# Gate logits of the first mixture: from split operands over the whole array to full-precision matmuls in four column groups

## Chip, cores, metric

One core of a Trainium2 chip runs the whole program. The metric is the device time in microseconds (us) of one execution; the median of three runs is compared. Five engines work side by side, each with its own stream of instructions, and meet only in semaphores: TensorE (PE; its weight loads are shown as PEld), VectorE (DVE), ScalarE (ACT), GpSimd (POOL) and SyncE (SP, which only issues DMAs here).

## What is computed

```python
# attention without softmax, decaying with distance; q, k, v are (4, 8, 576, 64)
scores = (1 / sqrt(64)) * q @ k.T
x = (scores * Dmat) @ v                 # Dmat[i, j] = gamma_h ** (i - j) for j <= i
x = x.transpose(...).reshape(2304, 512)
# first mixture: all 8 experts for every token, weights from Sinkhorn
logits = x @ w_gate                     # (2304, 8)
P = exp(logits - logits.max()), 8 rounds of row and column normalisation
x = sum_e P[:, e] * (relu(x @ w1[e]) @ w2[e])
# second mixture: each token goes to its best expert alone
out = gate_w * (relu(x @ w1b[best]) @ w2b[best])
```

The change concerns `logits = x @ w_gate` of the first mixture. All that matters of it lies in the first 112 us.

## The kernel before

**Attention (0 to 97 us).** 24 chunks, numbered `n = 0..23` (4 batches `b` of `NC = 6` chunks `c` of 96 positions). For each, TensorE runs in this order: the scores of the next chunk (L1373), the state update K'V (L1389, left out for the last chunk of a batch), the product with the state (L1399, left out for the first), and the masked scores times V (L1404). VectorE masks the scores (`PT`, L923), ScalarE copies the state (`ST`, L703) and the chunk's output (`Xf`, L708), GpSimd applies the decays (`QT` L527, `VD` L533), SyncE loads `QK` and `KV` of chunk `n + 6` as soon as chunk `n` is done. All of it is plain fp32, and a plain fp32 matmul stands as two MATMUL records in the trace, with a weight load each. The output of a chunk goes to bank 4 for even `c` and bank 0 for odd `c` (`OB`).

**Gates.** `x` transposed lies in three tiles `Xf`, each of two halves of `W = 384` tokens. Such a half has its logits made as soon as its tokens are there, six gates in all; `GATES` has for each the tile, the half and the chunk that completes it. For the first five, ScalarE rounds the half to fp32r (`GH`, L792, behind that chunk), VectorE forms the rest (`GL`, L956, one chunk later), and TensorE multiplies `WGA`/`WGB` with them in 8 fp32r matmuls that fill the 128 columns of the array and accumulate in bank `RB` (L1423, L1424, behind chunk `n + 2`). VectorE then transposes the 32x384 result into `LX` (L964). The sixth gate (`last_gate`, L1432) multiplies the unsplit `Xf` with `wgp` (32 columns) in four plain fp32 matmuls accumulated in one column group, in the first step of the mixture.

**First mixture (from 97 us).** 96 steps `k`. In each, TensorE makes the hidden layer by a Winograd-like scheme of 7 products `p0..p6` (6 fp32r matmuls each, L1447 to L1451) and the output of the step before (L1470 to L1472). Operands: `XH`/`XL` (halves of x or its differences `Tf`), written by ScalarE (`x_hi`, L737) and VectorE (`x_lo`, L949); `W1H`/`W1L` and `W2H`/`W2L` by ScalarE (L720, L724) and GpSimd (L560, L565), in the first steps partly VectorE (L992, L999). The weights of a step arrive in one buffer, `w1raw`, so the load of step 1 waits until step 0's has been split (`s_w1l`) and summed (`Sf`, L553, `s_sum`). VectorE adds partial sums (`c12`, `c22`, `c21`: L1168 to L1183), and each next product waits for one of them.

What stands in the program behind chunk 21 on VectorE is an order written by hand in the loop over `n`; each engine does strictly what is next in its own stream.

Of the kernel before, what the change touches and what calls it, by code (L numbers as in the profile page):

```python
# [90 lines left out]
def build(nc, qk, kv, wg1, w11, w12, wg2, w21, w22, attn_tab, keep_tab, gate_rows, out):  # L91
    ctx = ExitStack()
    with ctx:
# [70 lines left out]
        GH, _ = place("GH", [P, ND, W], F32R, at_x + 3 * 4 * NK * W)  # L164
        GL, _ = place("GL", [P, ND, W], F32R, at_x + 8 * 4 * NK * W)
        WGA, a = place("WGA", [P, ND, P], F32R, at_raw + 4 * 4 * 2 * P)
        WGB, a = place("WGB", [P, ND, P], F32R, a)
        assert a == at_w1b
# [42 lines left out]
        causal = atab[0:C, o:o + C]  # L211
        wgraw, a = place("wgraw", [P, ND, E], F32, a)
# [118 lines left out]
        s_wgz, s_wgh, s_gh, s_gl, s_gate, s_lgt = (sem(f"s_{x}") for x in ("wgz", "wgh", "gh", "gl", "gate", "lgt"))  # L331
# [19 lines left out]
        OB = (4, 0)  # L351
# [29 lines left out]
        def _(sp):  # L381
# [53 lines left out]
            sp.wait_ge(s_gate, NG - 1)  # L435
# [260 lines left out]
        def _(act):  # L696
# [88 lines left out]
            def gate_hi(g):  # L785

                sb, half, n = GATES[g]
                act.wait_ge(s_x, 2 + n + 1)
                if g > 0:
                    act.wait_ge(s_gate, g)  # L790
                for a in (0, 2):
                    nc.scalar.activation(GH[:, a:a + 2, :], Xf[sb][:, a:a + 2, half, :], ACT.Copy).then_inc(s_gh, 1)  # L792

            for n in range(B * NC):
                chunk(n // NC, n % NC)
                if n == 2:
                    act.wait_ge(s_wgz, 2)
                    act.wait_ge(s_wg1, 16)
                    for t in (WGA, WGB):
                        nc.scalar.activation(t[:, :, 0:E], wgraw[:, :, :], ACT.Copy).then_inc(s_wgh, 1)  # L800
                if n == 20:
                    w1_hi(0, 0, 0)
                    w1_hi(0, 0, 1)
                for g in range(NG - 1):
                    if n == GATES[g][2]:
                        gate_hi(g)
                if n in (14, 16, 18):
                    x_hi(0, n // 2 - 7)
                if n == 22:
                    w1_hi(0, 0, 2)  # L810
                    act.wait_ge(s_gate, NG - 1)
                    x_hi(0, 3)
                    x_hi(0, 4)

            def step(k, q, first=False, last=False, sb=0, route=None, late_x=None, scale=None, tile=None):
# [39 lines left out]
                for i in range(1, 4):  # L855
                    hidden_hi(k, i)

# [43 lines left out]
        def _(dve):  # L901
# [10 lines left out]
            for t in (WGA, WGB, wgp):  # L912
                nc.vector.memset(t[:, :, :].bitcast(F32), 0.0).then_inc(s_wgz, 1)
# [37 lines left out]
            def gate_lo(g):  # L951

                sb, half, _ = GATES[g]
                for i, a in enumerate((0, 2)):
                    dve.wait_ge(s_gh, 2 * g + i + 1)
# [12 lines left out]
            mask(0, 0)  # L968
            for n in range(B * NC):
                if n < B * NC - 1:  # L970
                    mask(n + 1, (n + 1) % NC)
                if n == 3:
                    dve.wait_ge(s_wgh, 2)
                    nc.vector.tensor_tensor(WGA[:, :, E:2 * E], wgraw[:, :, :], WGA[:, :, 0:E].bitcast(F32),
                                            ALU.subtract).then_inc(s_wgh, 1)
                    dve.wait_ge(s_wgz, 3)
                    nc.vector.tensor_copy(wgp[:, :, 0:E], wgraw[:, :, :]).then_inc(s_wgh, 1)
                for g in range(NG - 1):
                    if n == GATES[g][2] + 1:
                        gate_lo(g)  # L980
# [5 lines left out]
                if n in (15, 17, 19):  # L986
                    x_lo(0, (n - 15) // 2, s_xlp if n == 19 else s_xl)
# [15 lines left out]
            x_lo(0, 3, s_xlp)  # L1003
            x_lo(0, 4, s_xlp)
# [208 lines left out]
            def step(sb, k, e, q, **at):  # L1213
# [151 lines left out]
        def _(pe):  # L1365
# [48 lines left out]
            def gate(g):  # L1414

                sb, half, _ = GATES[g]
                if g == 0:
                    pe.wait_ge(s_wgh, 4)
                else:
                    pe.wait_ge(s_lgt, g * P // SQ)  # L1420
                pe.wait_ge(s_gl, 2 * g + 2)
# [3 lines left out]
                last.then_inc(s_gate, 1)  # L1425

            def last_gate():

                pe.wait_ge(s_lgt, (NG - 1) * P // SQ)
                sb, half, _ = GATES[NG - 1]  # L1430
                for a in range(ND):
                    last = mm(bank[RB][0:SQ, 0:W], wgp[:, a, :], Xf[sb][:, a, half, :],  # L1432
                              start=(a == 0), stop=(a == ND - 1))
# [7 lines left out]
            pe.wait_ge(s_x, 2 + B * NC)  # L1441
# [144 lines left out]
            for sb in range(SB):  # L1586
                for j in range(NQ if sb == 0 else PEEL * NQ):
# [3 lines left out]
                    if k == 0:  # L1591
                        after[7] = last_gate
# [105 lines left out]
```

## Time and profile before

| | us |
|---|---|
| median of 3 runs | 1906.84 (1906.82 to 1907.41) |
| the profiled execution | 1912.71 |
| its span, first to last instruction | 1911.1 |
| PE busy | 1887.9 (99%) |
| DVE busy | 1194.2 (62%) |
| POOL busy | 1085.7 (57%) |
| ACT busy | 633.5 (33%) |
| mean granted TensorE clock | 0.994 |

The profiled execution is 5.9 us above the median of the runs; differences between two places in the trace are taken as they are. A row of the timeline gives start, duration, engine, line, operation, tiles and shapes, how often it is repeated, and in square brackets how long the engine sat idle before and what ended that. Matmul durations include the pipeline, so what a matmul costs is read from one start to the next.

### The profile page before, as it was taken

What the parts mean: (1) busy time and instruction counts of PE and PEld (TensorE: products, weight loads), DVE (VectorE), ACT (ScalarE), POOL (GpSimd) and SP (SyncE); (2) the same over time, 40 slices, a digit from 0 to 9 for tenths busy, and PEclk for the clock granted to TensorE, in tenths of its full rate; (3) what the DMA queues carried; (4) which work ended last, traced back from release to release, by engine and by line L of the source; (5) the groups of instructions that cost most, each with busy time, mean ns of one, the idle gap of its engine ahead of it and who ended that gap; (6) DMA issues with size and microseconds to landing.
All of it is one profiled execution on the core that took longest, in us unless ns stands there. A gap on an engine that the chain in (4) does not pass through costs nothing.

```text
span 1911.1 us, 31124 instructions
## 1 busy us (share of the span) xinstructions
PE 1887.9 (99%) x11118; PEld 1709.1 (89%) x11118; DVE 1194.2 (62%) x2177; ACT 633.5 (33%) x1107; POOL 1085.7 (57%) x910
## 2 busy tenths in 40 slices
PE   8999999999999999999999999999999999999997
PEld 7889989999999999999999999999999999999997
DVE  4786765555567777775556777878666665322533
ACT  2543343333334333333333433333333332101221
POOL 5766666666678666666667876766666653111111
PEclk9999999999999999999999999999999998999999
DMA  9724444454444212122112122212222213312742
GB/s 232 185 95 149 155 155 155 148 165 158 153 161 140 67 67 83 67 83 66 66 66 78 66 78 74 87 67 78 78 99 99 88 61 122 138 35 67 266 175 69
DMA packets 123956, 212.16 MB, mean 111 GB/s; under 512 B 8974, under 2 KB 58126, under 8 KB 123856
## 3 DMA queue, kind: packets, MB, share of 16 engines
q1 hardware_dynamic: 118816, 195.31, 31.6%
q0 software_dynamic: 5040, 15.51, 2.4%
q8 instruction: 63, 1.03, 0.2%
q14 instruction: 37, 0.30, 0.1%
HBM read 162.65 MB, written 49.19 MB: 111 GB/s over the span
## 4 chain that ended last, share of the span: by engine, by line
PE 96%; DMA 1%; DVE 1%; issue 0%; SPq 0%; ACT 0%; POOL 0%; POOLq 0%; DVEq 0%; ACTq 0%
PE bank L1471 14%; PE bank L1472 14%; PE bank L1470 14%; PE bank L1447 12%; PE bank L1451 12%; PE bank L1449 12%; PE bank L1619 8%; PE bank L1629 2%; PE bank L1630 2%; PE bank L1631 2%; DMA wgraw<-in_moe_w_gate 1%; PE bank L1373 1%; PE bank L1404 1%; PE bank L1399 1%; PE bank L1583 1%; PE bank L1389 0%
## 5 line engine op out<-in xcount | busy, mean ns | idle before, releaser
L1210 DVE SCALAR_TENSOR_TENSOR acc<-bank,Pw,acc 128x512 f32<-128x512 f32 x516 | 386.1, 751 | 233.7 <-PE bank L1472 221.8
L1472 PE MATMUL bank<-W2H,HL 128*128 128x512 f32 x1152 | 450.1, 391 | 0.0
L1471 PE MATMUL bank<-W2L,HH 128*128 128x512 f32 x1152 | 450.0, 391 | 0.0
L1470 PE MATMUL bank<-W2H,HH 128*128 128x512 f32 x1152 | 449.2, 390 | 0.0
L560 POOL TENSOR_TENSOR W1L<-w1raw,W1H 128x512 fp32r<-128x512 f32 (+1 forms) x190 | 192.2, 1034 | 339.1 <-ACT W1H L720 339.1
L1447 PE MATMUL bank<-XHa,W1H 128*128 128x384 f32 x960 | 321.4, 335 | 2.0 <-DVE c L1183 1.1
L1451 PE MATMUL bank<-XHa,W1L 128*128 128x384 f32 x960 | 321.1, 334 | 0.0
L1449 PE MATMUL bank<-XLa,W1H 128*128 128x384 f32 x960 | 321.0, 334 | 0.0
L743 ACT ACTIVATE HH<-c 128x384 fp32r<-128x384 f32 x288 | 150.4, 526 | 489.5 <-PE bank L1472 324.5
L1472 PEld LDWEIGHTS bank<-W2H,HL 128*128 128x128 f32 x1152 | 216.2, 188 | 45.3
L1471 PEld LDWEIGHTS bank<-W2L,HH 128*128 128x128 f32 x1152 | 216.2, 188 | 42.8
L1470 PEld LDWEIGHTS bank<-W2H,HH 128*128 128x128 f32 x1152 | 216.3, 188 | 42.4
L565 POOL TENSOR_TENSOR W2L<-w2raw,W2H 128x1024 fp32r<-128x1024 f32 x96 | 230.5, 2402 | 27.2 <-ACT W2H L724 27.1
L560 POOL TENSOR_TENSOR W1L<-Sf,W1H 128x1024 fp32r<-128x1024 f32 x94 | 225.6, 2400 | 0.0
L553 POOL TENSOR_TENSOR Sf<-w1raw 128x256 f32<-128x256 f32 x192 | 147.7, 769 | 127.4 <-DMA w1raw<-in_moe_w 121.8
L743 ACT ACTIVATE HH<-bank 128x384 fp32r<-128x384 f32 x96 | 47.1, 491 | 447.7 <-PE bank L1472 447.7
L1188 DVE SCALAR_TENSOR_TENSOR HL<-c,HH 128x384 fp32r<-128x384 f32 x288 | 176.6, 620 | 11.0
L1447 PEld LDWEIGHTS bank<-XHa,W1H 128*128 128x128 f32 x960 | 180.2, 188 | 3.4 <-issue 1.7
L1451 PEld LDWEIGHTS bank<-XHa,W1L 128*128 128x128 f32 x960 | 180.2, 188 | 0.0
L1449 PEld LDWEIGHTS bank<-XLa,W1H 128*128 128x128 f32 x960 | 180.2, 188 | 0.0
L1619 PEld LDWEIGHTS bank<-x2T,Wa 128*128 128x128 f32 x1408 | 163.4, 194 | 1.9
L1619 PE MATMUL bank<-x2T,Wa 128*128 128x128 f32 x1408 | 164.3, 278 | 0.0
(198 smaller groups left out, 2616.6 us busy)
## 6 DMA issues: line engine op xcount, KB each, us to landing
w1raw<-in_moe_w SPq DMA_DIRECT2D x96, 512.0 KB
w2raw<-in_moe_w SPq DMA_DIRECT2D x96, 512.0 KB
sorted_rows<-blank SPq DMA_DIRECT2D x147, 257.0 KB, 3.7
Wa<-in_moe_w SPq DMA_DIRECT2D x7, 2048.0 KB, 7.5
Wb<-in_moe_w SPq DMA_DIRECT2D x7, 2048.0 KB, 9.8
QK<-qk SPq DMA_DIRECT2D x24, 384.0 KB, 8.4
KV<-kv SPq DMA_DIRECT2D x24, 384.0 KB, 9.7
nxt<-sorted_rows POOLq DMA_DIRECT2D x23, 257.0 KB
```

The lines of the kernel that those rows point to most:

```text
L560: nc.gpsimd.tensor_tensor(W1L[s][:, blk, :], raw, W1H[s][:, blk, :].bitcast(F32), ALU.subtract).then_inc(s_w1l, 1)
L565: nc.gpsimd.tensor_tensor(W2L[s][:, :, :], w2raw[:, :, :], W2H[s][:, :, :].bitcast(F32), ALU.subtract).then_inc(s_w2l, 1)
L743: nc.scalar.activation(HH[:, i, :], source, ACT.Relu).then_inc(s_hhi, 1)
L1188: nc.vector.scalar_tensor_tensor(HL[:, i, :], source, 0.0, HH[:, i, :].bitcast(F32), ALU.max, ALU.subtract).then_inc(s_hlo, 1)
L1210: ins = nc.vector.scalar_tensor_tensor(tile, psum, weight, tile, ALU.mult, ALU.add)
L1447: mm(bank[b][:, 0:W], W1H[s][:, blk, :], XH[i][:, c, :], start=start and c == 0, stop=False, skip_group_check=True)
L1449: mm(bank[b][:, 0:W], W1H[s][:, blk, :], XL[i][:, c, :], start=False, stop=False, skip_group_check=True)
L1451: last = mm(bank[b][:, 0:W], W1L[s][:, blk, :], XH[i][:, c, :], start=False, stop=(c == NK - 1), skip_group_check=True)
L1470: mm(dst, HH[:, h, tok], W2H[s][:, m, :], start=(m == 0), stop=False)
L1471: mm(dst, HH[:, h, tok], W2L[s][:, m, :], start=False, stop=False)
L1472: last = mm(dst, HL[:, h, tok], W2H[s][:, m, :], start=False, stop=(m == 1))
L1619: last = mm(bank[HB[j // 4]][:, (j % 4) * P:(j % 4 + 1) * P], Wa[s][:, a, j * P:(j + 1) * P], x2T[:, a, :], start=(a == 0), stop=(a == ND ...
```

## The change

The first five gates lose their split: no `GH`, `GL`, `WGA`, `WGB`. All six gates use the unsplit `Xf` and `wgp`, one plain fp32 matmul for each of the four blocks of 128 features, each into 32 partitions of its own of bank `RB`, so that each uses 32 of the array's columns. VectorE adds the four partial results: copies partitions 64 to 127 to `GS`, adds them onto 0 to 63, copies 32 to 63, adds them onto 0 to 31, each waiting for the one before, and then transposes as it did. For the last gate ScalarE makes the two copies (`GS_last`). The chunks' output banks are swapped, so that the last chunk writes bank 4, and TensorE no longer waits for its copy before the first product, which writes bank 0. The operand parts 3 and 4 of `x` are made behind chunks 19 and 21 instead of behind the loop. SyncE's load of the first `w2` no longer waits for the fifth gate.

```diff
-            OB = (4, 0)
+            OB = (0, 4)
@@ SyncE
-            sp.wait_ge(s_gate, NG - 1)
             load_w2(0, 0)
@@ ScalarE
-            def gate_hi(g): ...
-                    nc.scalar.activation(GH[:, a:a + 2, :], Xf[sb][:, a:a + 2, half, :], ACT.Copy).then_inc(s_gh, 1)
             for n in range(B * NC):
                 chunk(n // NC, n % NC)
...
-                if n in (14, 16, 18):
-                    x_hi(0, n // 2 - 7)
+                if n in (14, 16, 18, 19, 21):
+                    x_hi(0, (14, 16, 18, 19, 21).index(n))
                 if n == 22:
                     w1_hi(0, 0, 2)
-                    act.wait_ge(s_gate, NG - 1)
-                    x_hi(0, 3)
-                    x_hi(0, 4)
@@ ScalarE, step 0 of the mixture
                 for i in range(1, 4):
                     hidden_hi(k, i)
+                    if fixed(k, 0) and i == 1:
+                        act.wait_ge(s_gate, NG)
+                        nc.scalar.activation(GS_last[:, :], bank[RB][2 * SQ:P, 0:W], ACT.Copy).then_inc(s_gs, 1)
+                if fixed(k, 0):
+                    act.wait_ge(s_gsum, 1)
+                    nc.scalar.activation(GS_last[0:SQ, :], bank[RB][SQ:2 * SQ, 0:W], ACT.Copy).then_inc(s_gs, 1)
@@ VectorE
-            def gate_lo(g): ...
-                    nc.vector.tensor_tensor(GL[:, a:a + 2, :], Xf[sb][:, a:a + 2, half, :],
-                                            GH[:, a:a + 2, :].bitcast(F32), ALU.subtract).then_inc(s_gl, 1)
             def gate_tokens(g):
                 dve.wait_ge(s_gate, g + 1)
+                if g < NG - 1:
+                    link(nc.vector.tensor_copy(GS[:, :], bank[RB][2 * SQ:P, 0:W]))
+                    link(nc.vector.tensor_tensor(bank[RB][0:2 * SQ, 0:W], bank[RB][0:2 * SQ, 0:W], GS[:, :], ALU.add))
+                    link(nc.vector.tensor_copy(GS[0:SQ, :], bank[RB][SQ:2 * SQ, 0:W]))
+                    link(nc.vector.tensor_tensor(bank[RB][0:SQ, 0:W], bank[RB][0:SQ, 0:W], GS[0:SQ, :], ALU.add))
+                else:
+                    dve.wait_ge(s_gs, 2)
+                    link(nc.vector.tensor_tensor(bank[RB][0:SQ, 0:W], bank[RB][0:SQ, 0:W], GS_last[0:SQ, :],
+                                                 ALU.add))
...
-                if n in (15, 17, 19):
-                    x_lo(0, (n - 15) // 2, s_xlp if n == 19 else s_xl)
+                if n in (15, 17, 19, 20, 22):
+                    x_lo(0, (15, 17, 19, 20, 22).index(n), s_xl if n < 19 else s_xlp)
...
                     w1_sums_lo(1)
+                    dve.wait_ge(s_gs, 1)
+                    nc.vector.tensor_tensor(bank[RB][0:2 * SQ, 0:W], bank[RB][0:2 * SQ, 0:W], GS_last[:, :],
+                                            ALU.add).then_inc(s_gsum, 1)
@@ TensorE
             def gate(g):
...
                 for a in range(ND):
-                    mm(bank[RB][:, 0:W], WGA[:, a, :], GH[:, a, :], start=(a == 0), stop=False)
-                    last = mm(bank[RB][:, 0:W], WGB[:, a, :], GL[:, a, :], start=False, stop=(a == ND - 1))
+                    last = mm(bank[RB][SQ * a:SQ * a + SQ, 0:W], wgp[:, a, :], Xf[sb][:, a, half, :],
+                              start=True, stop=True)
                 last.then_inc(s_gate, 1)
...
-            pe.wait_ge(s_x, 2 + B * NC)
+            pe.wait_ge(s_x, 1 + B * NC)
```

VectorE's stream before, from the transposes of the fourth gate (behind the mask of chunk 21) to those of the fifth:

```order
L964 STREAM_TRANSPOSE LX<-bank 32x96 x4
L923 TENSOR_TENSOR PT_107<-bank,atab 96x384 x2
L956 TENSOR_TENSOR GL<-Xf_66,GH 128x768 x2
L992 TENSOR_TENSOR W1L_50<-w1raw,W1H_49 128x512
L992 TENSOR_TENSOR W1L_50<-w1raw,W1H_49 128x256
L923 TENSOR_TENSOR PT_109<-bank,atab 96x384 x2
L999 TENSOR_TENSOR W1L_50<-Sf,W1H_49 128x1024
L949 TENSOR_TENSOR XLa<-Xf_64,XHa 128x768
L949 TENSOR_TENSOR XLa<-Tf,XHa 128x768
L964 STREAM_TRANSPOSE LX<-bank 32x96 x4
```

The same stretch of VectorE's stream in the changed kernel (its own line numbers), from the fourth gate's sums on; those of the fifth gate stand behind the last row:

```order
L938 COPY GS<-bank 64x384
L939 TENSOR_TENSOR bank<-bank,GS 64x384
L940 COPY GS<-bank 32x384
L941 TENSOR_TENSOR bank<-bank,GS 32x384
L947 STREAM_TRANSPOSE LX<-bank 32x96 x4
L931 TENSOR_TENSOR XLa<-Xf_64,XHa 128x768
L905 TENSOR_TENSOR PT_104<-bank,atab 96x384 x2
L971 TENSOR_TENSOR W1L_50<-w1raw,W1H_49 128x512
L971 TENSOR_TENSOR W1L_50<-w1raw,W1H_49 128x256
L905 TENSOR_TENSOR PT_106<-bank,atab 96x384 x2
L931 TENSOR_TENSOR XLa<-Tf,XHa 128x768
L978 TENSOR_TENSOR W1L_50<-Sf,W1H_49 128x1024
```

The `GL` pair ahead of the first split of `w1raw` is gone; four sums stand ahead of the transposes, one operand part ahead of the mask of chunk 22 and one behind that of chunk 23.

VectorE's stream in step 0 of the mixture before, from the split of the weight sums of step 1 on:

```order
L999 TENSOR_TENSOR W1L_52<-Sf,W1H_51 128x1024
L1188 SCALAR_TENSOR_TENSOR HL<-c_75,HH 128x384
L1181 TENSOR_TENSOR c_74<-c_74,bank 128x384
L1183 TENSOR_TENSOR c_76<-cs_73,bank 128x384
L1188 SCALAR_TENSOR_TENSOR HL<-c_74,HH 128x384
```

The same place in the changed kernel:

```order
L978 TENSOR_TENSOR W1L_52<-Sf,W1H_51 128x1024
L1216 TENSOR_TENSOR bank<-bank,GS_last 64x384
L1165 SCALAR_TENSOR_TENSOR HL<-c_75,HH 128x384
L1158 TENSOR_TENSOR c_74<-c_74,bank 128x384
L1160 TENSOR_TENSOR c_76<-cs_73,bank 128x384
L1165 SCALAR_TENSOR_TENSOR HL<-c_74,HH 128x384
```

One sum of the last gate now stands between that split and `c21` (`c_76`).

## Rows read from the trace of the kernel before

**Rows 1.** The page's part 4, the chain that ended last.

```profile
PE 96%; DMA 1%; DVE 1%; issue 0%; SPq 0%; ACT 0%; POOL 0%; POOLq 0%; DVEq 0%; ACTq 0%
```

**Rows 2.** Waits of PE, 8 to 110 us: total, times, longest.

```profile
PE bank L1389 <- issue: 1.8, 2, 1.3
PE bank L1399 <- issue: 1.8, 2, 1.0
...
PE bank L1447 <- ACT Xf L708: 0.8, 1, 0.8
PE bank L1404 <- DVE PT L923: 0.4, 1, 0.4
```

**Rows 3.** Stretches between PE's stalls: length, PE busy (records), clock, DMA share, GB/s.

```profile
29.61:37.12 7.51, 7.51 (x127) 1.00 1.04 236
...
54.42:61.78 7.36, 7.34 (x126) 1.00 1.03 242
```

**Rows 4.** DMA queues, 29 to 63 us: packets, MB, share of the engines.

```profile
q8 instruction: 4, 0.07, 0.9%
```

**Rows 5.** Timeline of PE where it resumes after the first and the last such stall.

```profile
38.44 0.50 PE L1389 MATMUL bank<-VD,KV 96*64 96x64 f32 x9 [1.32 <-issue]
...
62.55 0.40 PE L1399 MATMUL bank<-QT,ST 64*64 64x96 f32 x5 [0.78 <-issue]
```

**Rows 6.** Timeline of PE: last product ahead of the third gate, its first matmul, what follows it.

```profile
69.06 0.88 PE L1404 MATMUL bank<-PT,VD 96*64 96x96 f32 x16
69.87 0.44 PE L1423 MATMUL bank<-GH,WGA 128*128 128x384 f32 x1
...
71.46 0.92 PE L1373 MATMUL bank<-QT,QK 64*96 64x96 f32 x16
```

**Rows 7.** Timeline of PE: the last gate, what follows, and step 1's second product.

```profile
103.16 2.77 PE L1432 MATMUL bank<-Xf,wgp 128*32 128x384 f32 x8
105.85 0.44 PE L1447 MATMUL bank<-XHb,W1H 128*128 128x384 f32 x1
...
110.02 0.41 PE L1447 MATMUL bank<-XHa,W1H 128*128 128x384 f32 x1 [0.76 <-DVE c L1183]
```

**Rows 8.** A stretch: length, PE, PEld, DVE, ACT, POOL busy, clock, DMA share, GB/s.

```profile
39.20:42.50 3.30, 3.30 (x40) 2.85 (x38) 0.00 (x0) 1.03 (x3) 1.00 (x2) 0.50 1.04 242
```

**Rows 9.** Timeline of DVE: two operations with a link behind, and a copy from a bank.

```profile
115.92 0.69 DVE L1204 COPY acc<-bank 128x512 f32<-128x512 f32 x1 [0.32 <-PE bank L1472]
...
129.74 0.32 DVE L1028 TENSOR_TENSOR bank<-bank,cs 128x144 f32<-128x144 f32 x1
130.09 0.32 DVE L1041 TENSOR_REDUCE bank<-bank 128x18 f32<-128x144 f32 x1
```

**Rows 10.** Timeline of DVE, 85 to 110 us.

```profile
85.76 1.18 DVE L964 STREAM_TRANSPOSE LX<-bank 32x96 f32<-32x96 f32 x4
...
89.15 2.88 DVE L956 TENSOR_TENSOR GL<-Xf,GH 128x768 fp32r<-128x768 f32 x2 [0.23 <-ACT GH L792]
91.96 3.09 DVE L992 TENSOR_TENSOR W1L<-w1raw,W1H 128x512 fp32r<-128x512 f32 x2
94.97 1.01 DVE L923 TENSOR_TENSOR PT<-bank,atab 96x384 f32<-96x384 f32 x2
...
97.90 0.95 DVE L949 TENSOR_TENSOR XLa<-Tf,XHa 128x768 fp32r<-128x768 f32 x1
...
105.33 3.15 DVE L999 TENSOR_TENSOR W1L<-Sf,W1H 128x1024 fp32r<-128x1024 f32 x1
...
109.33 0.54 DVE L1183 TENSOR_TENSOR c<-cs,bank 128x384 f32<-128x384 f32 x1
```

**Rows 11.** Timeline of POOL: step 0's last weight sum, step 1's first, its `W2L`.

```profile
93.59 1.18 POOL L553 TENSOR_TENSOR Sf<-w1raw,Sf 128x256 f32<-128x256 f32 x1
98.74 0.74 POOL L553 TENSOR_TENSOR Sf<-w1raw 128x256 f32<-128x256 f32 x1 [3.97 <-DMA w1raw<-in_moe_w]
...
105.01 2.39 POOL L565 TENSOR_TENSOR W2L<-w2raw,W2H 128x1024 fp32r<-128x1024 f32 x1
```

More of the change, by code:

```diff
@@ L163, in build @@
         assert 4 * 6 * D <= RSTEP and a + 4 * D <= at_h
[L164 to L168, printed above, removed]
+        GS, _ = place("GS", [2 * SQ, W], F32, at_c + 3 * 4 * W)
         KV, QK = [], []
@@ L211, in build @@
         causal = atab[0:C, o:o + C]
+        GS_last, g_end = place("GS_last", [2 * SQ, W], F32, a - 4 * attn_tab.shape[1])
+        assert g_end <= a
         wgraw, a = place("wgraw", [P, ND, E], F32, a)
@@ L330, in build @@
         s_dve = sem("s_dve")
-        s_wgz, s_wgh, s_gh, s_gl, s_gate, s_lgt = (sem(f"s_{x}") for x in ("wgz", "wgh", "gh", "gl", "gate", "lgt"))
+        s_wgz, s_wgh, s_gate, s_lgt, s_gs, s_gsum = (sem(f"s_{x}") for x in ("wgz", "wgh", "gate", "lgt", "gs", "gsum"))
         s_mx, s_gmx, s_nmx, s_exp = sem("s_mx"), sem("s_gmx"), sem("s_nmx"), sem("s_exp")
@@ L784, in _ @@
             act.wait_ge(s_x, 2)
[L785 to L791, printed above, removed]
-                    nc.scalar.activation(GH[:, a:a + 2, :], Xf[sb][:, a:a + 2, half, :], ACT.Copy).then_inc(s_gh, 1)
             for n in range(B * NC):
                 chunk(n // NC, n % NC)
[L796 to L800, printed above, removed]
                 if n == 20:
@@ L803, in _ @@
                     w1_hi(0, 0, 1)
-                for g in range(NG - 1):
-                    if n == GATES[g][2]:
-                        gate_hi(g)
-                if n in (14, 16, 18):
-                    x_hi(0, n // 2 - 7)
+                if n in (14, 16, 18, 19, 21):
+                    x_hi(0, (14, 16, 18, 19, 21).index(n))
                 if n == 22:
                     w1_hi(0, 0, 2)
-                    act.wait_ge(s_gate, NG - 1)
-                    x_hi(0, 3)
-                    x_hi(0, 4)
             def step(k, q, first=False, last=False, sb=0, route=None, late_x=None, scale=None, tile=None):
@@ L911, in _ @@
             nc.vector.memset(ST[0][:, 1, :], 0.0).then_inc(s_x, 1)
-            for t in (WGA, WGB, wgp):
-                nc.vector.memset(t[:, :, :].bitcast(F32), 0.0).then_inc(s_wgz, 1)
+            nc.vector.memset(wgp[:, :, :], 0.0).then_inc(s_wgz, 1)
             dve.wait_ge(s_atab, 16)
@@ L949, in x_lo @@
                 nc.vector.tensor_tensor(XL[i], part, XH[i].bitcast(F32), ALU.subtract).then_inc(done, 1)
[L951 to L955, printed above, removed]
-                    nc.vector.tensor_tensor(GL[:, a:a + 2, :], Xf[sb][:, a:a + 2, half, :],
-                                            GH[:, a:a + 2, :].bitcast(F32), ALU.subtract).then_inc(s_gl, 1)
             def gate_tokens(g):
@@ L972, in _ @@
                 if n == 3:
[L973 to L976, printed above, removed]
+                    dve.wait_ge(s_wgz, 1)
+                    dve.wait_ge(s_wg1, 16)
                     nc.vector.tensor_copy(wgp[:, :, 0:E], wgraw[:, :, :]).then_inc(s_wgh, 1)
                 for g in range(NG - 1):
-                    if n == GATES[g][2] + 1:
-                        gate_lo(g)
                     if n == GATES[g][2] + 3 and n < B * NC - 1:
@@ L1002, in _ @@
             w1_sums_lo(0)
-            x_lo(0, 3, s_xlp)
-            x_lo(0, 4, s_xlp)
             gate_tokens(NG - 2)
@@ L1414, in gate @@
             def gate(g):
-                sb, half, _ = GATES[g]
                 if g == 0:
-                    pe.wait_ge(s_wgh, 4)
+                    pe.wait_ge(s_wgh, 1)
                 else:
                     pe.wait_ge(s_lgt, g * P // SQ)
-                pe.wait_ge(s_gl, 2 * g + 2)
+                sb, half, n = GATES[g]
+                pe.wait_ge(s_x, 2 + n + 1)
                 for a in range(ND):
-                    mm(bank[RB][:, 0:W], WGA[:, a, :], GH[:, a, :], start=(a == 0), stop=False)
-                    last = mm(bank[RB][:, 0:W], WGB[:, a, :], GL[:, a, :], start=False, stop=(a == ND - 1))
[L1425 to L1433, printed above, removed]
+                    last = mm(bank[RB][SQ * a:SQ * a + SQ, 0:W], wgp[:, a, :], Xf[sb][:, a, half, :],
+                              start=True, stop=True)
                 last.then_inc(s_gate, 1)
@@ L1591, in _ @@
                     if k == 0:
-                        after[7] = last_gate
+                        after[7] = (lambda: gate(NG - 1))
                     if k == 1:
```

## The prediction, made before the changed kernel had run

> **What bounds the kernel now.** The chain that ended last is PE for 96% [rows 1]. So what the first 110 us gain or lose on PE shifts all the rest, and I ask only when PE passes a late point there: the second product of step 1, at 110.02 [rows 7]. The waits of PE say what holds it before that. The reader is to see that they are few: 1.8 and 1.8 us of "issue", 0.8 for the last chunk's copy, 0.4 for a mask [rows 2].
>
> The "issue" waits matter most. They cut a group of like matmuls in two (x9 and x5 are the remainders of groups of 16 [rows 5]), where the code has no wait. The stretches from one to the next hold 127 and 126 MATMUL records [rows 3], with as many weight loads some 256 instructions, whatever they are. The DMA queue "instruction" moved four packets in 29 to 63 us [rows 4], in which there are four such stalls (two of each line [rows 2]), while the engines of the DMA were at 1.03 to 1.04 [rows 3]. I read this as PE running out of instructions: the next 256 are asked for when the present ones begin, and come late behind the loads of QK and KV. Then up to 62.55 the pace is that of these fetches, and PE work saved inside such a stretch only lengthens its stall. After 62.55 there is no such stall.
>
> The other chain ends at `w1raw`. VectorE's `GL` (2.88 us from 89.15) stands ahead of its first split, which ends at 95.05 [rows 10]; then step 1's `w1raw` is loaded (POOL idle 3.97 us until 98.74 [rows 11]), summed, split, and after VectorE's split of the sums (105.33 to 108.48) and `c21` PE resumes at 110.02, having waited 0.76 [rows 7, 10].
>
> **The gate on PE.** Before, 8 fp32r matmuls: 71.46 - 69.87 = 1.59 us [rows 6]. After, 4 plain fp32 matmuls, 8 records. In one column group these 8 take 105.85 - 103.16 = 2.69, or 0.336 each [rows 7]: that is the upper bound. The masked product runs in two groups of 64 columns: 16 records of 96 columns would be 16 x 0.336 x 96/384 = 1.34 one after another, and took 69.87 - 69.06 = 0.81 [rows 6]. So two groups do overlap. With four at once two records' time is left, 0.67, and I add 0.11 for the change of form: 0.78, the lower bound. If they overlap only in pairs, four records' time: 1.45. I take 0.78, since nothing in the rows of two groups shows a limit. Saved per gate: 0.81; by pairs 0.14; without overlap 1.10 lost.
>
> The Trainium skill ("TensorEngine Tiling (Array Packing)", section Theoretical Speedup) gives up to 4 times for 32 columns, and the trace agrees for two groups. Its section PSUM Bottleneck on that page speaks against the change: after such a speedup the copy out of PSUM may become the bottleneck. By that rule VectorE's sums would set the pace; the terms for them follow from rows.
>
> **Which gates count.** Gates 0 (behind chunk 5) and 1 (behind chunk 11) lie before 62.55, in stretches that end in a stall; their 0.81 goes into it. Gates 2 and 3 lie behind: 2 x 0.81 = 1.62 sooner, everything from chunk 20 on. Call it X.
>
> **VectorE's sums.** A copy of 512 columns from a bank takes 0.69, an in-place multiply of 144 in a bank 0.32 [rows 9]: about 1.0 ns a column, so 384 columns 0.56. With a link the next starts 130.09 - 129.74 = 0.35 after a start, 0.03 over its duration. Four sums: 4 x 0.59 = 2.4 us. In front of the last mask (94.97 before) go 2.88 of `GL` and the idle time; what comes is 2.4 and one part of x (0.95, as the like row). Laid end to end from 85.76: sums to 88.2, transposes to 89.3, x part to 90.3, mask to 91.2, split of `w1raw` (3.03, of which I assume nothing is saved) to 94.2, mask to 95.2 [rows 10]. So the split ends 0.8 sooner than 95.05, besides X. Bounds for the four: 1.4 (0.35 each) and 2.8 (0.69 each); both keep the split ahead of POOL's sums, next.
>
> **The load of `w1raw`.** It needs VectorE's split and POOL's sums, which end at 94.77 [rows 11] and whose pace PE sets. So it comes at 94.8 - X, 0.3 better than X alone. The sums, splits and `W2L` behind it move along: `W2L`, which ended at 107.40, at 107.1 - X. VectorE's split of the sums took 3.15 and ended 1.08 after `W2L` [rows 10, 11], as if it got nowhere beside it; again it ends 1.08 behind, 108.2 - X. VectorE gets there in time even though the fifth gate's sums delay `c12` and `c22`: laid out as above its queue is free for it at 105.6 - X, with PE idle some 2.5 us in step 0. Here the last gate's shortening (2.69 to 0.78) goes: PE is sooner and waits longer.
>
> **The added sum ahead of `c21`.** 0.59, with nothing beside it, then as before 1.4 from the split's end (108.48) to `c21` (109.87) and 0.15 to PE: 110.3 - X. Against 110.02: +0.3 - 1.62 = -1.3.
>
> **At nothing.** ScalarE loses `GH` and gains two copies of about half a microsecond behind work that PE needs only eight matmul groups later. The first product no longer waits 0.8 for the last chunk's copy [rows 2]; it starts sooner, and the time is spent again at 110. The parts 3 and 4 of x on ScalarE lie in its idle time. The load of `w2` stands in SP's queue behind `w1raw`'s, which is issued after the fifth gate anyway. Without that cover each would cost up to its own 0.5 to 1 us.
>
> **Sum.** Against its own execution 1912.7 - 1.3 = 1911.4 (span 1909.8). The median of the runs is 5.9 lower, so 1906.84 - 1.3 = 1905.5.
>
> **Rivals.**
> *The clock falls.* After the 1.32 us stall before 38.44 the granted clock was 0.50 over 39.20 to 42.50, 1.2 instead of 2.4 GHz [rows 5, 8]; after the stalls of 1.0 and 0.78 it stayed at 1.00 [rows 2, 3]. The change lengthens idle time: the stall before 62.55 from 0.78 to 1.6, and PE now has 2.5 in step 0 and about 2 before 110, in place of 0.76. A fall costs half of 3.3 us, 1.65, where PE is the bound: one gives 1907.2, two 1908.8. Three, or one that lasts longer, give 1910.4 and more: slower. The point to pass is one more stall as long as the 1.32 us after which it fell. For it: the stalls grow beyond that. Against it: part of the slow time lies ahead of waits and is hidden.
> *Full saving.* If the "issue" stalls are not fetches, gates 0 and 1 count too: -2.9, 1903.9; if the fall at 39.2 also goes, 1902.3, faster. Against it: the 127, 127 pattern.
> *No overlap, or in pairs.* Column groups of one bank, with four moving operands of 128 rows, may share a path. In pairs X = 0.3: 1906.8. Not at all: gates 2 and 3 lose 2.2, gate 1 its 1.1 less the 0.8 stall: X = -2.5, 1909.6. Two groups overlapping speaks against it.
> *The change does nothing here*, as the gates' saving and VectorE's cost cancel: 1906.8, no other than pairs.
>
> **How the numbers follow.** A measurement of this kernel tells about 0.2%, 3.8 us, from no change: below 1903.0 is faster, over 1910.7 slower. Chances: the sum 0.34; one or two falls 0.25; three or a long one (slower) 0.10; full saving 0.09, with more than that (faster) 0.10; pairs or none 0.12, of which 0.03 slower with a fall. So faster 0.10, same 0.77, slower 0.13. The range leaves out the slower tail and the fastest: 1903.0 to 1909.8.
>
> **What would show it.** Right: a gate of 0.7 to 0.9 us from start to start; no `GH`/`GL`; still stalls each 127 records up to about 62.5, the ones before 38.4 and 62.5 longer by 0.8; four sums at 0.59; PE idle over 1.5 us before the second product of step 1, now near 108.7, on `c21`. Wrong: scores of chunk 17 sooner by more than 0.8, a gate over 1.2, a clock of 0.50 anywhere in 60 to 115, or PE waiting for a mask more than 0.5 us.

## The result, and the profile after

| us | before | after |
|---|---|---|
| median (six runs each) | 1906.83 (1901.57 to 1907.79) | 1914.01 (1912.61 to 1918.18) |
| the profiled execution, span | 1912.71, 1911.1 | 1913.54, 1911.9 |

After against before: 1.0039, interval [1.0023, 1.0054]: slower, by some 7 us, and above the predicted range. The same kernel run again later gave 1.0049 [1.0036, 1.0063]. The two profiled executions differ by only 0.8 us, so a single pair of traces would have hidden the result: before's happens to be 6 us above its median, after's is at its own. The two were also 2.7 us apart before the first gate ran, after the same work on PE: the masked product ahead of it starts at 28.56 in after and at 31.27 in before, whose early waits are 1.1 us longer (5.6 against 4.5 us from 8 to 28 us) and which has a stretch at half clock there. That part of after's lead is no effect of the change. Three lines of before: its longest wait, that stretch (0.50 is the clock), and the product.

```profile
PE bank L1373 <- POOL QT L527: 4.3, 2, 3.4
...
11.80:15.20 3.40, 3.40 (x46) 3.10 (x48) 0.87 (x2) 2.32 (x4) 1.99 (x2) 0.50 1.03 230
...
31.27 0.88 PE L1404 MATMUL bank<-PT,VD 96*64 96x96 f32 x16
```

The page of after. PE has less to do (1882.2 against 1887.9) and is yet later.

```profile
PE 1882.2 (98%) x11118; PEld 1700.8 (89%) x11118; DVE 1195.0 (63%) x2186; ACT 627.1 (33%) x1097; POOL 1086.0 (57%) x910
...
PE 95%; DVE 2%; POOL 1%; issue 1%; DMA 1%; ACT 0%; SPq 0%; POOLq 0%; DVEq 0%; ACTq 0%
```

The waits of PE in after, 8 to 111 us (total, times, longest); they answer to [rows 2]. The copy of the last chunk is gone from the list. New are 3.7 us on `c21` (L1160) and 2.3 for a mask (L905).

```profile
PE bank L1419 <- DVE c L1160: 3.7, 1, 3.7
PE bank L1353 <- POOL QT L524: 2.8, 2, 2.5
PE bank L1384 <- DVE PT L905: 2.6, 2, 2.3
PE bank L1369 <- issue: 1.7, 2, 1.0
PE bank L1419 <- DVE c L1151: 1.4, 1, 1.4
PE bank L1353 <- issue: 1.2, 1, 1.2
```

The timeline of PE in after: the second gate with what follows it, then the place where PE waits for the mask of chunk 14, and the third gate.

```profile
49.42 0.85 PE L1404 MATMUL bank<-Xf,wgp 128*32 128x384 f32 x8
50.20 0.92 PE L1353 MATMUL bank<-QT,QK 64*96 64x96 f32 x16
...
60.33 1.39 PE L1384 MATMUL bank<-PT,VD 96*64 96x96 f32 x14 [2.33 <-DVE PT L905]
...
67.34 1.51 PE L1404 MATMUL bank<-Xf,wgp 128*32 128x384 f32 x8
68.78 1.43 PE L1353 MATMUL bank<-QT,QK 64*96 64x96 f32 x16
```

A gate takes 50.20 - 49.42 = 0.78 us, as predicted. The third takes 1.44, because it ran at half the clock, as these stretches of after show (length, busy times, clock, DMA share, GB/s):

```profile
59.60:69.80 10.20, 9.47 (x100) 7.28 (x102) 3.49 (x7) 2.47 (x5) 4.00 (x4) 0.50 0.58 167
110.80:114.20 3.40, 3.40 (x13) 3.40 (x12) 2.88 (x8) 3.35 (x7) 2.58 (x3) 0.51 0.00 0
121.10:124.50 3.40, 3.40 (x10) 2.63 (x9) 1.02 (x3) 0.25 (x1) 1.42 (x3) 0.50 0.00 0
```

Why the mask is late stands in VectorE's timeline of after, just ahead:

```profile
51.43 1.01 DVE L905 TENSOR_TENSOR PT<-bank,atab 96x384 f32<-96x384 f32 x2
52.46 0.56 DVE L938 COPY GS<-bank 64x384 f32<-64x384 f32 x1
...
54.82 1.19 DVE L947 STREAM_TRANSPOSE LX<-bank 32x96 f32<-32x96 f32 x4
56.04 1.59 DVE L924 TENSOR_TENSOR Tf<-Xf 128x768 f32<-128x768 f32 x1
57.55 1.79 DVE L924 TENSOR_TENSOR Tf<-Xf,Tf 128x768 f32<-128x768 f32 x1
59.27 1.94 DVE L905 TENSOR_TENSOR PT<-bank,atab 96x384 f32<-96x384 f32 x4
```

Between two masks stand four sums (54.82 - 52.46 = 2.36 us), four transposes and two differences `Tf`: 59.27 - 52.46 = 6.8 us. PE idles 2.33 us for the second mask, and from 59.6 to 69.8 the granted clock is 0.50. In before the same place took 63.22 - 59.37 = 3.85 us:

```profile
59.37 1.18 DVE L964 STREAM_TRANSPOSE LX<-bank 32x96 f32<-32x96 f32 x4
...
63.22 1.01 DVE L923 TENSOR_TENSOR PT<-bank,atab 96x384 f32<-96x384 f32 x2
```

VectorE and GpSimd of after around step 1's second product; they answer to [rows 10, 11].

```profile
97.97 0.74 POOL L550 TENSOR_TENSOR Sf<-w1raw 128x256 f32<-128x256 f32 x1 [5.22 <-DMA w1raw<-in_moe_w]
...
104.44 2.38 POOL L562 TENSOR_TENSOR W2L<-w2raw,W2H 128x1024 fp32r<-128x1024 f32 x1 [0.18 <-ACT W2H L721]
...
114.68 2.39 POOL L562 TENSOR_TENSOR W2L<-w2raw,W2H 128x1024 fp32r<-128x1024 f32 x1 [0.22 <-ACT W2H L721]
117.03 2.42 POOL L557 TENSOR_TENSOR W1L<-Sf,W1H 128x1024 fp32r<-128x1024 f32 x1
```

```profile
105.25 2.66 DVE L978 TENSOR_TENSOR W1L<-Sf,W1H 128x1024 fp32r<-128x1024 f32 x1
107.83 0.55 DVE L1216 TENSOR_TENSOR bank<-bank,GS_last 64x384 f32<-64x384 f32 x1
108.30 1.08 DVE L1165 SCALAR_TENSOR_TENSOR HL<-c,HH 128x384 fp32r<-128x384 f32 x1
109.30 0.54 DVE L1158 TENSOR_TENSOR c<-c,bank 128x384 f32<-128x384 f32 x1
109.77 0.54 DVE L1160 TENSOR_TENSOR c<-cs,bank 128x384 f32<-128x384 f32 x1
...
114.79 2.45 DVE L989 TENSOR_TENSOR lg<-LX 128x144 f32<-128x144 f32 x1
117.27 0.30 DVE L990 TENSOR_REDUCE mx<-lg 128x1 f32<-128x144 f32 x1
117.61 1.92 DVE L991 TENSOR_SCALAR diag<-ktab,mx 128x128 f32<-128x128 f32 x1
```

PE of after at the same place: the second product of step 1, and the `diag` matmul.

```profile
110.45 0.41 PE L1419 MATMUL bank<-XHa,W1H 128*128 128x384 f32 x1 [3.69 <-DVE c L1160]
...
119.58 0.49 PE L1504 MATMUL bank<-diag,ktab 128*128 128x128 f32 x2 [1.77 <-DVE diag L991]
```

The same three operations in before, ahead of GpSimd's `W2L` or just clear of it:

```profile
113.55 0.31 DVE L1012 TENSOR_TENSOR lg<-LX 128x144 f32<-128x144 f32 x1
...
114.23 0.32 DVE L1014 TENSOR_SCALAR diag<-ktab,mx 128x128 f32<-128x128 f32 x1
```

```profile
114.49 2.41 POOL L565 TENSOR_TENSOR W2L<-w2raw,W2H 128x1024 fp32r<-128x1024 f32 x1
```

The second product starts at 110.45 against 110.02: 0.4 later, though the first product started 4.3 sooner (93.43 against 97.75). From there on: 1.7 us for the clock at 110.8, 1.77 of wait for `diag`, 1.7 for the clock at 121.1; with the 0.4 that is 5.6 us. The shift measured is 5.4: one and the same VectorE operation, the 1500th from the end, starts at 1078.11 and at 1072.72. Near 1609 before's profile has 10.2 us at half the clock, with PE busy and not one wait, which after's lacks, and 0.8 is left at the end.

**How the clock is weighed over many runs.** Each timed run lists its span and its mean granted clock; span x (1 - clock) is the time lost at half clock. As a mean over the runs it is 7.3 to 8.0 us for before (four sets of 23 to 35 runs) and 13.1 and 14.1 for after (6 and 6). Span x clock, the time at full clock, is 1896.6 to 1897.2 against 1900.0 and 1900.4. So 5 to 7 us of the loss are clock and some 3 are not. I call the first "clock loss" below. The scatter of the runs leaves such a mean uncertain by some 0.5 us for a set of before, 1 for twelve runs and up to 2 for five or six, so differences of 1 to 2 us in it mean little.

### The profile page after: what moved, and what is told of

The parts are those of the page before. It is cut to its first block, busy times and chain, and to the rows that moved or that the text cites. A ratio compares the mean times of both kernels' runs of the same rounds, so it can differ in the third digit from the quotient of the medians.

```text
span 1911.9 us, 31121 instructions
## 1 busy us (share of the span) xinstructions
PE 1882.2 (98%) x11118; PEld 1700.8 (89%) x11118; DVE 1195.0 (63%) x2186; ACT 627.1 (33%) x1097; POOL 1086.0 (57%) x910
## 4 chain that ended last, share of the span: by engine, by line
PE 95%; DVE 2%; POOL 1%; issue 1%; DMA 1%; ACT 0%; SPq 0%; POOLq 0%; DVEq 0%; ACTq 0%
PE bank L1443 14%; PE bank L1444 14%; PE bank L1442 14%; PE bank L1419 12%; PE bank L1423 12%; PE bank L1421 12%; PE bank L1591 8%; PE bank L1602 2%; PE bank L1601 2%; PE bank L1603 2%; PE bank L1384 1%; PE bank L1353 1%; PE bank L1379 1%; PE bank L1555 1%; PE bank L1369 0%
```

## The experiments

All are timed against the kernel before on the same chip; each ratio is against it. Where two variants are compared with each other, some 3 us (0.15%) is what their intervals leave open. Not one leaves out part of the computation; some add work whose result is not used.

**The last gate as before.** After, but with the old `last_gate` (one column group) and no sums for it.

```diff
-    mm(bank[RB][SQ * a:SQ * a + SQ, 0:W], wgp[:, a, :], ..., start=True, stop=True)
+    mm(bank[RB][0:SQ, 0:W], wgp[:, a, :], ..., start=(a == 0), stop=(a == ND - 1))
... (without the copies to GS_last on ScalarE and its sums on VectorE)
```

> The changed kernel, but with the last gate as before: four matmuls accumulated in one column group (2.69 us of PE), no copies by ScalarE and no sums by VectorE for it. Theory A (the loss is made in steps 0 and 1: VectorE's added sums push c21 and the diagonal behind GpSimd's operations, PE idles 3.7 and 1.8 us, and the clock falls to half twice): the wait for the diagonal (1.77) goes, the wait ahead of step 1's second product shrinks from 3.69 to about 1.8 less 0.6, at most one fall is left, and the time is 1914.0 less 4 to 5.5: 1908.5 to 1910, or 1907 with no fall at all. Theory B (the loss comes from the attention stage: the 2.33 us wait for a mask and the 10 us at half clock behind it): no gain, 1913 to 1915.

1911.28, 1.0029 [1.0017, 1.0041]; clock loss 13.2, full-clock time 1896.6. No wait for `diag`, 2.7 us on `c21`, still 2.3 for the mask. The time lies between what the two theories wanted. So the last gate holds perhaps 2.7 us, within what the intervals leave open, and the larger part is elsewhere.

**The diagonal later.** After, with TensorE's `diag` matmuls two output groups on.

```diff
-                        after["t0"] = diagonal
+                        after["t2"] = diagonal
```

> The changed kernel, with the matmul on the diagonal issued behind the third output tile of step 1 instead of the first. Theory A: PE no longer waits 1.77 us there, and the fall of the clock behind that wait (3.4 us at half, 1.7 us lost) goes with it: 1914.0 - 3.5 = 1910.5. Theory B (attention stage): 1914. If only the wait goes and the clock falls all the same: 1912.3.

1914.17, 1.0046 [1.0033, 1.0059]. The wait for `diag` is gone from the profile, the full-clock time is 1896.2, but the clock loss is 16.5: nothing won, against theory A.

**Filling the wait.** After, with 16 matmuls (results unused) ahead of step 1's second product.

```diff
+                    if fixed(k, 1):
+                        for i in range(16):
+                            mm(bank[7][:, 0:W], W1H[s][:, 0, :], XH[0][:, 0, :], start=True, stop=True)
```

> The changed kernel, with 16 matmuls more (128x384, fp32r, about 2.8 us, results unused, in a bank that is free) behind the first product of step 1, where PE waits 3.69 us for c21. They add work inside a wait. If the clock falls at 110.8 because PE idled before it (theory A), the wait shrinks to about 0.9, the clock stays at full speed there, and the time falls by 1.7: 1912.3, with the second wait for the diagonal unchanged or up to 1.7 longer, since PE is there sooner. If idling has nothing to do with the fall: 1914.

1913.38, 1.0042 [1.0029, 1.0056]; clock loss 11.1. PE waits 0.9 in place of 3.7 and its profile has no fall at 110 and one alone, of 3.4 us, at 60.2. But this profile is of the quickest of the five runs (1906.74; the others 1912.37 to 1915.73), and the median is what it was. That the falls behind 110 cost nothing is not shown by it, as five runs would not show 1.7 us.

**The late mask removed.** After, with the third and fourth difference `Tf` one chunk later, so that they no longer stand with the second gate's sums ahead of one mask.

```diff
-                if n in (11, 12):
-                    x_term(0, 2 * n - 22)
-                    x_term(0, 2 * n - 21)
+                if n in (11, 13):
+                    x_term(0, n - 11)
+                    x_term(0, n - 10)
```

> The changed kernel, with VectorE's third and fourth difference of x moved from behind chunk 12's place in its stream to behind chunk 13's, so that the mask of chunk 14 does not stand behind them and the second gate's four sums. Theory A: PE's wait of 2.33 us at 58 and the 10.2 us at half clock behind it go, PE is at the mixture up to 5 us sooner, and the whole comes out at 1913 to 1914 all the same, because the load of the weights of step 1 hangs on the landing of those of step 0 and PE waits longer. Theory B: 1914.0 less up to 7: 1907 to 1909.

1909.81, 1.0019 [1.0007, 1.0032]; clock loss 11.1: 4.2 us given back, the largest effect of one edit. PE no longer waits there, and no fall of the clock stands between 43 and 107 us in the profile. Theory A, no gain, is out. VectorE there, with a mask now between transposes and differences:

```profile
57.21 1.19 DVE L947 STREAM_TRANSPOSE LX<-bank 32x96 f32<-32x96 f32 x4
58.43 1.02 DVE L905 TENSOR_TENSOR PT<-bank,atab 96x384 f32<-96x384 f32 x2
59.37 0.95 DVE L924 TENSOR_TENSOR Tf<-Xf 128x768 f32<-128x768 f32 x1
60.23 0.95 DVE L924 TENSOR_TENSOR Tf<-Xf,Tf 128x768 f32<-128x768 f32 x1
61.10 1.01 DVE L905 TENSOR_TENSOR PT<-bank,atab 96x384 f32<-96x384 f32 x2
```

**Both.** The last gate as before and the late mask removed.

> The changed kernel with both of the single edits: last gate as before (4.0 to 2.7 us better than the change in the runs so far) and VectorE's differences of x one chunk later (4.2 us better). If the two losses are separate (the mask wait with its falls of the clock; the last gate's sums ahead of c21 and the diagonal): 1914.0 - 2.7 - 4.2 = 1907.1, no difference from before that can be told. If they are one and the same loss met twice (falls of the clock that come wherever PE idles): 1909 to 1911, with a mean clock still under that of before.

1906.80, 1.0003 [0.9991, 1.0015]; clock loss 9.1, full-clock time 1896.0. The two effects add up (1914.0 - 2.7 - 4.2 = 1907.1), and with them the whole loss is gone, with the first five gates still in column groups. Against the kernel with the old last gate alone the late mask is worth 1911.3 - 1906.8 = 4.5. Nothing is won either, as far as can be told: the 1.3 us that I had predicted lie inside this interval.

**Single parts, from the kernel before.** Only the banks swapped, and only the first five gates in column groups (sums with them, the parts of `x` where they were, SyncE's wait gone). The edit of the first:

```diff
-            OB = (4, 0)
+            OB = (0, 4)
-            pe.wait_ge(s_x, 2 + B * NC)
+            pe.wait_ge(s_x, 1 + B * NC)
```

> The kernel before, with only the output banks swapped and the wait for the last chunk's copy gone. PE starts the mixture 0.8 us sooner and waits 0.8 us longer for c21 of step 0, which hangs on the weights' load: theory A (the load chain sets the end of step 0) 1906, unchanged. If PE set it: 1905.1. If the longer wait there already brings a fall of the clock: 1907.7.

> The kernel before, with only the first five gates changed (full precision, four column groups, VectorE's four sums) and SyncE's wait for them gone; last gate, banks and the operand parts 3 and 4 as before. Theory A2 (the gates' sums make the mask of chunk 14 late, PE waits 2.3 us and the clock falls; the mixture's part of the loss is the last gate's): about 4 us over before, 1910, with a mean clock lower than before by about 0.002. If the loss is all in the last gate and the moved parts: 1905 to 1906.

Banks: 1906.38, 1.0006 [0.9992, 1.0019]. The first product starts without its 0.8, and PE waits 2.2 for `c21` in place of 0.76: spent again, as predicted. Gates alone: 1909.04, 1.0026 [1.0013, 1.0038], clock loss 10.8, with 2.3 us for the mask. So the early gates carry half of the loss or more (1.0026 of 1.0039 to 1.0049), with the late mask in the profile.

**The load of `w1raw` alone.** "Both", with SyncE holding the loads of `ktab`, `w2` and `wg2s` back until step 1's `w1raw` has landed.

```diff
             load_w1(0, 1)
+            sp.wait_ge(s_w1raw, 32)
```

> The kernel of both edits (e5), and SyncE issues the loads of the table, of w2 and of the second gate's weights only when step 1's w1 has landed. In the changed kernel that w1 landed 5.2 us after its issue, before 3.6. If the loads issued behind it took its share: 3.6 or less again, the whole chain to step 1's second product 1.5 us sooner, 1.5 us under e5. If it was something else (the instruction fetch of PE, which runs in the same time): 5.2 as before and no gain, or up to 1 us worse where w2 is now late.

1907.39, 1.0014 [1.0002, 1.0027]. GpSimd waits for it as long as in after:

```profile
95.62 0.74 POOL L551 TENSOR_TENSOR Sf<-w1raw 128x256 f32<-128x256 f32 x1 [5.17 <-DMA w1raw<-in_moe_w]
```

It is not the loads behind it that make this one 5.2 us where [rows 11] has 3.97. Nor is it an accident of one profile: from SyncE's issue to GpSimd's first sum this load took 3.4 to 3.9 us in the seven profiles with the old early gates and 4.4 to 5.5 in the eleven with early gates in column groups.

**The late mask put into the kernel before.** Seven copies of 64x384 (results unused) on VectorE ahead of the second gate's transposes. Nothing else is changed: fp32r gates, no column groups for the first five. The copies take 4.15 us, more than the four sums, and make PE's wait as long as in after.

```diff
                 dve.wait_ge(s_gate, g + 1)
+                if g == 1:
+                    for i in range(7):
+                        link(nc.vector.tensor_copy(GS[:, :], bank[RB][2 * SQ:P, 0:W]))
```

> The kernel before, with seven copies more on VectorE (0.59 us each, 4.1 in all, results unused) ahead of the transposes of the second gate, so that the mask of chunk 14 comes as late as in the gates-only kernel (PE waits about 2.3 us for it); no column groups but the last gate's one. If a late mask alone makes the loss, with the falls of the clock that it brings: 1909 to 1910, span x (1 - clock) 2 to 4 us over that of before. If PE makes up for the wait because the load chain sets the end of the attention stage anyway, and the column groups are what lets the clock fall: 1906 to 1907, clock as before.

1911.38, 1.0030 [1.0018, 1.0041]: clock loss 11.9 against 7.4 of before, full-clock time 1897.8 against 1897.2. The timeline of PE, then the stretch behind it:

```profile
65.32 1.55 PE L1408 MATMUL bank<-PT,VD 96*64 96x96 f32 x16 [2.49 <-DVE PT L924]
```

```profile
64.70:74.90 10.20, 9.58 (x88) 8.47 (x88) 5.11 (x9) 2.47 (x5) 6.26 (x4) 0.50 0.62 172
```

The loss is the one of "gates alone", without an early gate in column groups. The wait of 2.5 us goes with 10.2 us at 0.50, here as in after; 4.5 of the 5.3 us lost are clock.

The stretch is not always that long. Seven profiles have this wait, of 2.33 or 2.49 us, and each has a stretch at half clock that begins between 0.7 us before its end and 1.0 behind: 10.2 us in three (after, this one, the diagonal later), 6.8 in "gates alone", 3.4 in the other three. Two of them, "gates alone" and after again:

```profile
63.30:70.10 6.80, 6.80 (x80) 6.04 (x80) 2.75 (x5) 1.98 (x4) 2.00 (x2) 0.50 0.58 168
...
73.30:76.70 3.40, 3.40 (x46) 3.11 (x47) 1.88 (x3) 1.94 (x4) 2.00 (x2) 0.50 0.66 230
```

**Controls, and filling once more.** The kernel before as one of the kernels tried, "both" with 12 of the filling matmuls, and after again:

> The kernel before, unchanged, as one of the timed ones: 1906, ratio 1.000 within 0.0015. Its profile shows how far two executions of one program differ in the first 112 us: the falls of the clock elsewhere or none, and the first product of the mixture within 3 us of 97.75.

> The kernel of both edits (e5) with 12 matmuls (128x384, fp32r, about 2.1 us, results unused) in the wait for c21 of step 0 (2.1 us in e5). If idling there costs falls of the clock: span x (1 - clock) down by 1 us or more from 9.05 and 1905.5. If not: 1906.8 as e5; if the matmuls end after c21: up to 1 us more.

> The changed kernel, unchanged, on the same chip as the others: 1912 to 1914, ratio 1.003 to 1.0045, the mask wait of 2.3 us and the waits for c21 (3 to 4 us) and for the diagonal (about 1 to 2 us) in its profile again, the falls of the clock at other places.

1.0002 [0.9990, 1.0014], 1.0009 [0.9996, 1.0021] and 1.0049 [1.0036, 1.0063]. Filling the 2.1 us wait of "both" wins nothing that can be told. After again is slower than I expected (1916.86, 1.0049), and before again had its first product at 93.92, not within 3 us of 97.75.

**What the last gate costs.** The kernel before with one unused copy of 64x384 (0.55 us) on VectorE, at two places: ahead of `hidden_lo(k, 1)`, where after has its added sum, or ahead of `lg`. The first place also with the diagonal later.

```diff
                     w1_sums_lo(1)
+                    dve.wait_ge(s_gate, NG)
+                    nc.vector.tensor_copy(GSX[:, :], bank[RB][0:2 * SQ, 0:W])
                 hidden_lo(k, 1)
```

```diff
+                link(nc.vector.tensor_copy(GSX[:, :], bank[RB][0:2 * SQ, 0:W]))
                 link(nc.vector.tensor_tensor(lg[:, :, :], ...))
```

> The kernel before with one copy of 64x384 from the gates' bank on VectorE (0.55 to 0.59 us, its result unused) where the changed kernel has its added sum, ahead of the second hidden part of step 0. Theory A (the added sum costs by itself and by moving lg and diag behind the W2L of GpSimd): second product of step 1 0.5 later, lg at about 114.1 on the scale of the kernel before, diag beside W2L, TensorE waits 1 to 2 us for it, and idle time brings falls of the clock: ratio 1.0015 to 1.003. Rival B (what the last gate costs lies in the clock falls after the 3.7 us of idle time that its shortening makes, not in the sum): within 0.0005 of the kernel before.

> The kernel before with the same unused copy later, between the last gate's transposes and lg, so that the second product of step 1 is untouched. Theory A: lg starts at about 114.1, diag near 114.8 beside the W2L of GpSimd and ends 2 us late; TensorE waits up to 1.8 us for it: ratio 1.001 to 1.0015. Rival B: the diagonal has slack, TensorE waits less than 0.3: 1.0000.

> The unused copy of the first of these runs, with TensorE's diagonal put two output groups later (it stands behind t2, not t0), so that only the sum itself is left. Theory A: 0.5 us and no wait for the diagonal: 1.0002 to 1.0005. Rival B: the same as the first of these runs.

1.0004 [0.9988, 1.0019], 0.9998 [0.9981, 1.0014] and 1.0002 [0.9987, 1.0017]. The mechanism is there; the timeline of VectorE in the second of them, and PE's wait:

```profile
109.41 0.36 DVE L1014 TENSOR_TENSOR lg<-LX 128x144 f32<-128x144 f32 x1
...
110.14 2.08 DVE L1016 TENSOR_SCALAR diag<-ktab,mx 128x128 f32<-128x128 f32 x1
```

```profile
PE bank L1534 <- DVE diag L1016: 1.2, 1, 1.2
```

In the first, PE waits 1.7 for `c21` in place of 0.76, and 0.3 for `diag`. All three results agree with a cost of what PE waits, 1 us, and with none: these intervals cannot tell the two apart. My theory A for the first (1.0015 to 1.003) was too high, and the first result is what rival B wanted.

**After without its two late operations.** The late mask removed and the diagonal later, last gate as in after.

> The changed kernel with the two Tf differences one chunk later and the diagonal two output groups later, its last gate as it is. Theory A: the late mask gone gives 4.2 back and the diagonal's wait 1.8 of the other 2.7: 1.0003 to 1.0012. Rival B (the 3.7 us of idle time before the second product is what costs, through the clock): as with the Tf differences alone, 1.0019.

1910.69, 1.0013 [0.9996, 1.0031]; clock loss 11.3, full-clock time 1895.8. It agrees with both theories: the interval holds 1.0003 to 1.0012 as well as 1.0019. Its full-clock time is 1 us below before's, its clock loss 4 above, and PE still waits 3.7 for `c21`.

## Why the prediction was wrong

**Right.** The gate: 0.78 us predicted, 0.78 measured. The Trainium skill ("TensorEngine Tiling (Array Packing)", section Theoretical Speedup) gives up to 4 times for 32 columns; the trace has 2.69 / 0.78 = 3.4 for plain fp32 matmuls, so it agrees with that bound. The sums: 0.59 each, start to start. VectorE's split of the sums ending 1.08 behind GpSimd's `W2L`: 107.91 - 106.82 = 1.09. The banks worth nothing. PE idle twice in step 0 (0.8 + 1.4 where I had 2.5) and before `c21` (3.7, longer than my 2).

**The step that failed: "VectorE's sums".** I laid VectorE's row end to end only where `GL` stood, from 85.76 on, and put the sums at nothing everywhere else, without a reason. Behind chunk 12 they are not free: the second gate's sums come with four transposes and two differences `Tf`, and the mask of chunk 14 is queued behind all of them. I named "PE waiting for a mask more than 0.5 us" as a sign of error without pricing it. Shown by experiments from both sides: the mask moved ahead of the differences gives 4.2 of the 7 us back (4.5 with the last gate as before), and a wait as long put into the kernel before costs 1.0030. The Trainium skill ("TensorEngine Tiling (Array Packing)", section PSUM Bottleneck), which I had named and not followed beyond the last masks, says that after such a speedup the copy out of PSUM may become the bottleneck. The trace agrees at one place, this wait of 2.33 us.

**The rival "the clock falls" was mis-sized, not wrong.** I gave 0.10 to three falls or a long one. The clock loss rose by 5 to 7 us over the runs. A fall in the rows is not always 3.4 us long: around a wait of 2.33 or 2.49 it was 3.4 to 10.2, which costs 1.7 to 5.1. The wait itself seems to have been largely caught up (4.5 of the 5.3 us of the late mask in before are clock). The Trainium skill ("TensorE: Matmul & The Clock Gate", section HAM oscillation) tells of a kernel in which DMA waits of some 3 to 5 us between groups of matmuls throw the clock back to half each time. The traces agree in kind, for shorter waits: it fell around all seven of 2.33 or 2.49 us. Priced at 10.2 us, the late mask alone brings my 1905.5 to 1910.6, the edge of my slower side.

**The chain to `c21`.** Predicted 1.3 sooner, measured 0.4 later. Three terms. PE was further ahead than X: 4.3 at the first product, but 2.7 of it is the lead from before the first gate and 0.8 the bank. Counted from the first gate the second product is 81.1 us away, against 77.9 in before: 3.1 later. The load of `w1raw`, issued 92.78 against 95.13, was waited for 5.22 us in place of 3.97, and the sums and splits behind it took longer (97.97 to 106.82, 8.9, against 98.74 to 107.40, 8.7), so `W2L` ended 0.6 sooner, where I had 0.3 + 1.6. And `HL` behind the added sum took 1.08 where before had 0.55, beside GpSimd's `Sf`: from the split's end to that of `c21` 110.31 - 107.91 = 2.4 us, where before had 1.4 and I had added 0.59. The 5.2 us are not explained: the loads behind were excluded, and they come with the early gates in column groups, as shown above. In after a packet of PE's instruction queue lands in that stretch and in before it does not, but "banks" has one there too with 3.9 us and "gates alone" none with 4.4, so it is not that alone; the cause stays open.

**Gates 0 and 1.** I put their 0.81 into the instruction stalls, two of which were to grow by it. They did not: from 28 to 63 us after has two (0.96 before 34.54, 0.78 before 41.76) where before has four with 3.6 in total [rows 2], and the stretches between them are shorter (34.54 to 41.76 is 7.2 us; before 46.95 to 54.43, 7.5, and 38.44 to 46.95, partly at half clock, 8.5). So the pace up to 62 us is not that of the fetches alone. How much PE gained by this can't be read from one pair: from the first gate to the first product the kernel before took 65.7 us in one profile and 63.8 in another, after 64.1 and 66.5. In reading [rows 2] I had also passed over its longest waits, 4.3 us for GpSimd's `QT` and 1.3 for ScalarE's `ST`; both lie before 28 us, and no sum of mine rests on them.

**The last gate.** Undoing it gives 2.7 us beside after, and 3.0 beside the kernel without the late mask (1909.8 against 1906.8). Two steps that I had missed are shown to exist: the added sum makes PE wait 1 us more, and it moves `lg` and `diag` beside GpSimd's two long operations, where they take 2.45 and 1.92 us. Each alone is worth about 1 us and can't be told from nothing.

The profiles show a third step, the clock behind the longer wait on `c21`. From step 1's second product to the 1500th VectorE operation from the end, the profiles of the kernels with the last gate in column groups take 963.9 to 967.7 us (six of them, 967.7 in after), and those with the old last gate 962.1 to 962.8, but for the late `lg` (963.6) and the banks alone (963.8, with a fall at 108.7). Where PE waited 3.3 to 3.7 us for `c21`, five profiles, 3.4 or 6.8 us at half clock stood around or right behind it each time; where it waited 2.1 to 2.7, in one of four; where it waited less, in none of nine, and that holds the filled wait. So a gate made 1.9 us shorter by column groups turned into idle time, and the idle time went with a fall. That this, the added sum and `diag` make up all of 2.7, and why the diagonal put later won nothing in the median of after, stays open.

## What to carry to other kernels

Lay out the row of every engine at each place where an operation is added, not only where the change is meant to act: what counts is how much stands between two operations that the bound engine waits for (6.8 us against a chunk of about 3), not the engine's mean load. Price a new wait of TensorE above 2 us with the clock around it, by the range of stretches at half clock that the profiles have (3.4 to 10.2 us here), not by the shortest. Where a kernel's gain is hidden behind a chain, undoing the parts one by one against many runs tells more than two traces: here the two profiled executions were 0.8 us apart and the kernels 7. Before comparing two traces, find the first place that the change touches, and count from there: here they were already 2.7 us apart.

## What the hardware showed that I had not expected

- Small VectorE operations that start behind the start of a long GpSimd `tensor_tensor` end 0.1 to 0.2 us behind its end: `lg` 0.31 or 2.45 us, `diag` 0.32 or 1.92 to 2.08. `HL` took 0.55 or 1.08, beside a shorter one; copies and sums with an operand in a bank kept 0.55 (the last gate's second sum at 112.98, beside `W1L`). The Trainium skill ("Advanced Engine Details and Errata", section VectorE Performance Modes) says that VectorE's second SBUF port is shared with GpSimd, so that VectorE's 2-port instructions and GpSimd's block each other. It gives `tensor_scalar` such a mode and `tensor_tensor` none. The row of `diag`, a `tensor_scalar`, agrees; that of `lg`, a `tensor_tensor`, is slowed as much, beyond what the section says.
- Stretches at half clock are not all behind waits: the kernel before has one of 10.2 us near 1605 in two of its profiles, "both" has it too, with PE busy for all of it and no wait in the 20 us ahead. Just ahead stand matmuls with 8 moving columns (`wg2s`), 8 records in 0.8 us.
- Filling a wait with matmuls did not make the kernel faster in the median, for 3.7 us in after and for 2.1 in "both"; the profile of the first has no fall behind the filled wait.
